# An expert layer tile by tile on TensorE: where each step's waits and table read stand, and how the last, conditional steps are written

## The reference

```python
def _moe2_ref(x, w_gate, w_local, w1, w2):
    ...
    for b in range(B):
        prev_e = -1
        for s in range(S):
            fresh_e = int(np.argmax(logits[b, s]))
            if s == 0 or local_gate[b, s] < 0.5:
                e = fresh_e
            else:
                e = prev_e if prev_e >= 0 else fresh_e
            prev_e = e
            ...
            h = np.maximum(x[b, s] @ w1[e], 0.0)
            out[b, s] = p[e] * (h @ w2[e])
```

## Time and profile before

| | |
|---|---|
| median of three runs | 875.97 us |
| lowest, highest | 875.25, 876.46 us |
| the profiled execution | 875.92 us |
| its span | 874.1 us |
| TensorE busy | 838.1 us, 96% of the span |
| VectorE busy | 406.3 us, 46% |
| ScalarE busy | 339.4 us, 39% |
| GpSimd busy | 245.5 us, 28% |
| chain that ended last | TensorE 89%, VectorE 3%, "issue" 3% |

### The profile page before, as it was taken

The page is one execution under the profiler, slowest core; times in us unless marked ns, Lnnn a source line. Parts: engine busy times, 40 slices in busy tenths (PEclk is TensorE's granted clock), DMA queues, the critical chain, the costliest instruction groups (busy, mean ns, idle before and its releaser), DMA issues.

```text
span 874.1 us, 19838 instructions
## 1 busy us (share of the span) xinstructions
PE 838.1 (96%) x7380; PEld 725.0 (83%) x7381; DVE 406.3 (46%) x731; ACT 339.4 (39%) x752; POOL 245.5 (28%) x288
## 2 busy tenths in 40 slices
PE   7899999999999999999999999999999999999995
PEld 6898989799899997899988989897777777777773
DVE  4677778411255255335447635626854324322111
ACT  4677776411155145226315514523324324222210
POOL 5977877792000000000000000085341121122121
PEclk9999999999999999999999999999999999999998
DMA  6553452148222021002101205125143313110110
GB/s 161 144 141 106 119 138 70 51 145 0 25 84 62 1 73 49 25 37 68 41 34 51 60 1 208 58 93 208 49 146 121 139 48 126 36 48 31 35 49 31
DMA packets 36173, 68.01 MB, mean 78 GB/s; under 512 B 11352, under 2 KB 11480, under 8 KB 36120
## 3 DMA queue, kind: packets, MB, share of 16 engines
q1 hardware_dynamic: 26168, 44.90, 19.0%
q10 hardware_dynamic: 6512, 11.64, 4.5%
q0 software_dynamic: 3440, 10.75, 3.8%
HBM read 57.84 MB, written 9.98 MB: 78 GB/s over the span
## 4 chain that ended last, share of the span: by engine, by line
PE 89%; DVE 3%; issue 3%; POOL 2%; ACT 2%; ACTq 0%; POOLq 0%; DVEq 0%
PE bank L1743 23%; PE bank L1745 23%; PE bank L1744 22%; PE bank L1683 4%; PE bank L1628 4%; PE bank L1653 4%; PE bank L1638 1%; PE bank L1960 1%; PE bank L1790 1%; PE bank L1616 1%; PE bank L1819 1%; PE bank L1669 1%; DVE stage L1206 1%; ACT stage L1011 1%; PE bank L1947 1%
## 5 line engine op out<-in xcount | busy, mean ns | idle before, releaser
L1175 DVE SCALAR_TENSOR_TENSOR hid_lo<-bank,hid_hi 128x384 fp32r<-128x384 f32 x96 | 53.5, 557 | 210.0 <-ACT hid_hi L987 210.0
L1745 PE MATMUL bank<-uT_hi,W 128*128 128x384 f32 x384 | 129.6, 337 | 0.0
L1743 PE MATMUL bank<-uT_hi,W 128*128 128x384 f32 x384 | 129.4, 337 | 0.0
L1744 PE MATMUL bank<-uT_lo,W 128*128 128x384 f32 x384 | 128.9, 336 | 0.0
L987 ACT ACTIVATE hid_hi<-bank 128x384 fp32r<-128x384 f32 x96 | 46.9, 488 | 186.8 <-PE bank L1745 186.7
L1011 ACT ACTIVATE stage<-stage 128x512 f32<-128x512 f32 x135 | 84.5, 627 | 77.3 <-DVE stage L1206 70.8
L1743 PE MATMUL bank<-W,hid_hi 128*128 128x512 f32 x288 | 114.0, 396 | 0.3 <-DVE hid_lo L1175 0.3
L1745 PE MATMUL bank<-W,hid_lo 128*128 128x512 f32 x288 | 113.7, 395 | 0.0
L1744 PE MATMUL bank<-W,hid_hi 128*128 128x512 f32 x288 | 113.4, 394 | 0.0
L1206 DVE TENSOR_TENSOR stage<-rows,stage 128x512 f32<-128x512 f32 x135 | 89.0, 687 | 11.0 <-ACT stage L1011 8.5
L1456 DVE TENSOR_TENSOR stage<-bank,slot_p 128x512 f32<-128x512 f32 x20 | 13.8, 692 | 144.2 <-PE bank L1745 144.2
(11 more groups left out here) (305 smaller groups left out, 1545.7 us busy)
## 6 DMA issues: line engine op xcount, KB each, us to landing
rows<-in_moe_w SPq DMA_DIRECT2D x12, 1024.0 KB, 5.1
stage<-gate_rows ACTq DMA_DIRECT2D x38, 256.0 KB, 3.2
stage<-in_moe_w_ch SPq DMA_DIRECT2D x16, 512.0 KB, 3.9
qk_raw<-in_q SPq DMA_DIRECT2D x32, 144.0 KB, 3.4
vv<-in_v SPq DMA_DIRECT2D x32, 144.0 KB, 2.8
x_rows<-rows SPq DMA_DIRECT2D x6, 768.0 KB, 3.2
qk_raw<-in_k SPq DMA_DIRECT2D x30, 144.0 KB, 3.6
late_stage<-in_moe_w SPq DMA_DIRECT2D x4, 1024.0 KB, 6.7
```

The costliest lines, as they stand in the source:

```text
L1175: dve.scalar_tensor_tensor(out=hid_lo[:, n % 2], in0=bank[:, HB[n % 2], 0:TOK], scalar=0.0, in1=hid_hi[:, n % 2].bitcast(F32), op0=ALU.max ...
L1743: pe.matmul(dst, lhs_hi, rhs_hi, start=start, stop=False)
L1744: pe.matmul(dst, lhs_hi, rhs_lo, start=False, stop=False)
L1745: return pe.matmul(dst, lhs_lo, rhs_hi, start=False, stop=stop)
```

## The change

`sure_steps` is split out of `expert_steps`; ScalarE, VectorE and GpSimd keep the same order as before. On TensorE `step(i)` now begins with its table read and all its waits (the weights, `h_out`, and by `x_ready` the gathered rows of tile i+1 and their place), one `settled`, then turns `hrow` of tile i-1 and the rows of tile i+1, and then runs the up products of tile i and the down products of tile i-1. Step 3 has no turns of its own; six chunks of tile 2's down products are run before it instead of four, two of them behind the turn of tile 4's rows. The steps from 18 on are written out one inside the `If` of the other, so that the first that fails leaves them all. Behind them stand the last turns and the last down products.

```diff
@@ -439,12 +439,15 @@
-        def expert_steps(eng, step):
-            end = load_last(eng)
+        def sure_steps(eng, step):
             step(EARLY_T + 1, 1)
             with eng.Fori(EARLY_T // 2 + 1, FULL // 2) as n:
                 step(2 * n, 0)
                 step(2 * n + 1, 1)
+
+        def expert_steps(eng, step):
+            end = load_last(eng)
+            sure_steps(eng, step)
...
             def turn_x_halves(i):
-                pe.wait_ge(gathered, 16 * i)
-                pe.wait_ge(xT_out, i)
-                settled(pe)
...
             def turn_h_halves(i, g):
-                if g == 0:
-                    pe.wait_ge(h_out, 2 * i + 2)
-                else:
-                    pe.wait_ge(xT_out, i + 2)
-                settled(pe)
...
+            def x_ready(i):
+                pe.wait_ge(gathered, 16 * i)
+                pe.wait_ge(xT_out, i)
+
             def step(i, x_par):
-                own_ = of_tile(i)
-                up_start(i, *own_, x_par)
-                up_part(own_[0], 1, range(KC), x_par)
-                if isinstance(i, int):
-                    down_part(i - 1, 0, range(4, NEC))
+                par, ord_ = of_tile(i)
+                pe.wait_ge(ew_lo, 2 * EP * ord_ + EP)
+                if not (isinstance(i, int) and i == EARLY_T + 1):
+                    pe.wait_ge(h_out, 2 * i)
+                    x_ready(i + 1)
+                    settled(pe)
+                    turn_h_halves(i - 1, 0)
+                    turn_h_halves(i - 1, 1)
+                    turn_x_halves(i + 1)
+                up_part(par, 0, range(KC), x_par)
+                up_part(par, 1, range(KC), x_par)
+                if isinstance(i, int) and i == EARLY_T + 1:
+                    down_part(i - 1, 0, range(6, NEC))
                 else:
                     down_start(i - 1, *of_tile(i - 1), range(NEC))
-                turn_h_halves(i, 0)
-                turn_h_halves(i, 1)
-                turn_x_halves(i + 2)
-
+
+            def last_steps(i):
+                if i < TILES:
+                    with pe.If(end >= i):
+                        step(i, i % 2)
+                        last_steps(i + 1)
...
             down_part(2, 0, range(2, 4))
+            x_ready(4)
+            settled(pe)
             turn_x_halves(4)
+            down_part(2, 0, range(4, 6))
             pe.wait_ge(tables_ready, 1)
-            end = expert_steps(pe, step)
-            down_start(end, *of_tile(end), range(NEC))
+            end = load_last(pe)
+            sure_steps(pe, step)
+            last_steps(FULL)
+            par, ord_ = of_tile(end)
+            pe.wait_ge(ew_lo, 2 * EP * ord_ + 2 * EP)
+            pe.wait_ge(h_out, 2 * end + 2)
+            x_ready(end + 2)
+            settled(pe)
+            turn_h_halves(end, 0)
+            turn_h_halves(end, 1)
+            turn_x_halves(end + 2)
+            pe.wait_ge(y_out, end)
+            down_part(end, par, range(NEC))
```

## The result

The changed kernel takes 861.15 us, median of four runs (860.10 to 862.48), against 876.06 us for the kernel before in the same measurement (875.25 to 876.46). The ratio is 0.983, 95% interval 0.9815 to 0.9849. It is faster, by 14.9 us; 20.9 us were forecast. The median lies 2.2 us above the range of the prediction. The profiled execution took 861.76 us, with a span of 859.9 us.

The account below looks back on a forecast made before the run. TensorE was taken to be bound by its sequencer's uncovered work behind short turns. Gains of 14.9 (boundaries), 1.3 (entry), 3.0 (end) and 1.7 (clock) sum to 20.9 us: 875.92 to 855.0 us, range 853.0 to 859.0.

Parts of the forecast that it names:

- What bounds the kernel: Expert stage: TensorE's pauses are its sequencer's own work, uncovered behind short turns; 12.5 us in 16 pauses.
- The boundaries: 16 boundaries, steps 4 to 19: pauses vanish once the table read is covered; gain 14.9 us, ends 12.5 and 16.5.
- The extra of 0.15 us a boundary: Product behind 64-row turns starts before their modelled end; 0.15 us at each of 16 boundaries, between nothing and 0.25.
- The entry: Before step 3: six down products run inside the 1.36 us of idle time; gain 1.3 us, between 1.0 and 1.4.
- The end: Last down products: wait for `hT_lo` alone, gain 3.0 us; no clock fall, gain 1.7 us.
- The term for the jump: Branch leaving the nest over six steps: bounds 0.2 and 6.8 us, taken as no cost.
- The far jump misses: Rival, leaving the nest: last turns up to 3.9 us late, clock may fall, 1.7; price 1 to 5.5 us; chance 0.10.
- the four faster cases: Forecast as summed 0.76, jump 0.10, issue behind the turns 0.08, lead lost 0.04; faster was given as 0.96.
- still under cover: Jump out of the nest: at least one code packet must be fetched, hidden under 4.1 us, so the sum stays.
- issue fast enough: Rival denied here: first product behind the turns 0.25 us late at every boundary, 4 us, 859.0; chance 0.08.
- the lead was there: Rival denied here: waits ahead of the turns hold the sequencer, so pauses only move; about 870 us; chance 0.04.
- the late gather: Rival: gathered rows, now awaited ahead of all turns, land too late in the steps; slower, 878 us; chance 0.02.

Follow-up runs that it names:

- e5_nest24: The changed kernel with its nest written out only to step 23, so the jump out passes over four steps (760 instructions): 856.50 us, ratio 0.978.
- e5_nest25: The changed kernel with its nest written out only to step 24, so the jump out passes over five steps (950 instructions): 856.10 us, ratio 0.9773.
- e8_pad_dead: The changed kernel with 30 never-executed matmuls in the innermost If, moving the code behind the nest 60 instructions further on: 856.97 us, ratio 0.9783.
- e1: The changed kernel with last turns and last down products written once per possible last tile, ahead of the far jump: 856.05 us, ratio 0.978.
- e2: The changed kernel with the last steps in a loop of two Ifs a round instead of nested: 857.22 us, ratio 0.979.
- e4: The kernel before, step order untouched, with only the last steps nested: 874.49 us, ratio 0.9988.
- e7: The kernel before with two more chunks of tile 2's down products run before step 3: 875.39 us against 875.73, ratio 0.9998.

## Why the prediction was wrong

**What bounds the kernel: right.** The pauses were the sequencer's own work, and they left when it was given cover; the lead of 4.1 us read from the register operation at 657.0 is what the table read has now, 4.0 us.

**The boundaries: right mechanism, one term too large.** The 12.5 us of pauses all went. The extra of 0.15 us a boundary was taken between nothing and the 0.25 that the earlier trace rows show behind full turns; it is 0.07 in the row at 660.04, and the whole comes to 0.84 us a boundary instead of 0.93. That is 1.5 us. The cause is not the register operations: at the entry the down product at 638.59 has fixed addresses and starts just 0.07 us before the modelled end of the half turns (638.66), too.

**The entry: right,** 1.3 for 1.3.

**The end: the step that failed.** "No row shows a jump that far. Its bounds: 0.2 us, and two fetches one after the other", and then "I take nothing, since 1.2 us for a packet is the row that is nearest." The packet's time was the wrong row. A jump out of the held code took 3.3 to 3.9 us in every run that has one. The packet itself took 0.93 to 1.44 us of that, which fits the 1.2 us that the prediction read; what the term left out is the 1.0 us from branch to packet and the 1.4 us from packet to the next instruction, and the nearest row for the whole was the other one that stood there, the 3.3 us from issue to landing. Even so this first fetch would have done no harm: e5_nest24, e5_nest25 and e8_pad_dead all have it and end at 856 to 857 us. The harm came from the second, a break of 1.96 us, which falls behind the cover because the turns, not the products, are what is being issued then. The term for the jump was put at nothing; the end came out 5.1 us short of its forecast (4.7 and -0.4), and 4.9 of these are the difference to e1, where nothing waits for the jump. From the place where the last turns should start to the first product it is 4.9 us in the changed kernel (840.34 to 845.23) and 2.2 in e1 (838.48 to 840.66): 2.7 us of delay. Of the 4.9 us by which the two differ to the end of the span, the other 2.2 us are products at the lower clock, which held for 6.8 us.

**The rival named it.** "The far jump misses" had this mechanism, both fetches and the clock, and a price of 1 to 5.5 us; 5.1 was found. It was given 0.10. Its middle of 3 us was too low, and the upper end of the range, 859.0, left out its own end of 860.5 (and 3.9 and 1.7 make 5.6, not 5.5). Even that is 0.65 us below the median; the rest is within the shortfall at the boundaries. The chances of the four faster cases also sum to 0.98, not to 0.96. The Trainium skill, "Runtime: NRT & Kernel Launch", section "Instruction fetch mechanics", says that a taken branch to a page outside those held waits for a fetch. The traces agree: seven kernels have such a branch, it took 3.3 us or more in all, and one packet of code arrived in each. The argument for "still under cover" counted one fetch; the last 24 turns with their weight loads are 48 instructions, and here the place where a second fetch is needed fell among them.

**The other rivals** fell by the rows: no pause stands behind the turns (issue fast enough), the lead was there, and the late gather came near but did not matter. The gather beside the weight loads again took 7.2 us at the longest: issued at 675.18, it landed 0.9 us before the turns at 683.27.

**The version to use** is e1: it is written out for every number of tiles, and at 856.05 us beats the changed kernel by 4 to 5 us and the kernel before by 20 us (2.2%). By time it cannot be told from e2, which serves every number of tiles with less code. How either fares where another number of tiles is needed no run shows.

## What to carry to other kernels

Put a sequencer's slow work (table reads, waits that are met anyway, branches) behind long products, not behind short ones; cover is the sum of what is queued, here about 4 us of products but less than 1 us of turns. A far jump is a wait for code, and a second wait can follow it: take it after the last instruction that anyone waits for, or write the steps so that only short jumps are needed. Price an operation that no row shows at the bad end when another engine or the clock hangs on it.

## What the runs showed of the hardware

- A branch out of the code at hand stopped TensorE's sequencer for 3.33 to 3.91 us (seven kernels, over 760 instructions and more), against 0.36 us over 190 and 0.2 us over one step before. Of that, 1.0 us passed before a packet of 16 KB started, 0.93 to 1.44 us were the packet, and 1.4 us passed behind it. Soon after it, the changed kernel stopped a second time, for 1.96 and 1.69 us in its two traces, until 1.4 us after the next packet; 60 instructions of code that never runs moved that away.
- Half turns (64 rows) are followed by a product 0.07 us before their modelled end, full turns 0.25 us before.
- With a pause of 4.2 us the granted clock was at its lower level for about 3.4 us in one trace (before: 0.57 over 4 us) and for some 6.8 us in two others (e4 and e7: 0.52 and 0.50 over 4 us, then 0.63 and 0.66 over 4); after idle pieces of 0.41 and 1.96 us in the changed kernel it was there for 6.8 us (0.50). With pauses of up to 1.26 us ahead of the last products it stayed at 1.00 under them.
